# Linear attention with two soft-routed expert layers: VectorE's order in the first chunks, and the first weight loads in pieces of 512 KB

## The reference

```
# attention, per head: B=4, H=8, S=768, D=64
for t in range(S):
    state = gamma * state + outer(k[t], v[t])
    y[t] = scale * (q[t] @ state)
x = y as (3072, 512)                       # N = 3072 tokens, 512 wide
# soft MoE: 8 experts, 4 slots each, F = 1024
logits = x @ phi                           # (N, 32)
d = softmax(logits, axis=0); c = softmax(logits, axis=1)
slot_out[e] = relu((d.T @ x)[e] @ w1[e]) @ w2[e]
x = c @ slot_out
# top-2 MoE, noisy gates
noisy = x @ w_gate + log1p(exp(x @ w_noise)) * noise
out[token] = sum over its two best experts of weight * relu(x @ w1[e]) @ w2[e]
```

## Time and profile before

| | |
|---|---|
| median of 3 runs | 549.07 us (546.41 to 551.51) |
| profiled execution | 547.3 us |
| its span | 545.6 us |
| mean granted TensorE clock | 0.969 |
| PE busy | 496.7 us (91%) |
| DVE busy | 277.1 us (51%) |
| attention, from the start to the first product with w1a | 132.16 us |

### The profile page before, as it was taken

One profiled execution on the slowest core, in us unless ns is written; L12 is line 12 of the kernel. 1 busy time (PEld: TensorE's weight loads), 2 busy tenths in 40 slices (PEclk: granted clock), 3 DMA queues, 4 the chain that ended last, 5 costly groups with the idle time before them and its releaser, 6 DMA issues.

```text
span 545.6 us, 13537 instructions
## 1 busy us (share of the span) xinstructions
PE 496.7 (91%) x4845; PEld 294.6 (54%) x4846; DVE 277.1 (51%) x449; ACT 185.3 (34%) x345; POOL 257.9 (47%) x216
## 2 busy tenths in 40 slices
PE   4898989997977568799999999999999999999995
PEld 4686777873476344345545455454554545545452
DVE  1775757565411698573564645454646242332422
ACT  0121222222000835773645544536352222322210
POOL 1222221212000016455686868686887766656543
PEclk9999999998997688899999999999999999999998
DMA  7999999988999999415554452123232343333410
GB/s 274 358 353 417 373 379 389 336 337 305 420 424 426 403 414 380 165 51 193 188 191 136 125 179 55 30 52 52 36 59 43 47 57 44 47 50 41 55 24 1
DMA packets 32358, 107.91 MB, mean 198 GB/s; under 512 B 11567, under 2 KB 12831, under 8 KB 27840
## 3 DMA queue, kind: packets, MB, share of 16 engines
q1 hardware_dynamic: 18144, 92.89, 44.0%
q0 software_dynamic: 14176, 14.49, 14.7%
HBM read 93.87 MB, written 29.43 MB: 226 GB/s over the span
## 4 chain that ended last, share of the span: by engine, by line
PE 81%; DMA 7%; DVE 6%; issue 3%; ACT 1%; POOL 1%; SPq 0%; DVEq 0%; POOLq 0%
PE ps L988 51%; PE ps L971 5%; PE ps L655 4%; PE ps L719 4%; DMA late_w1a<-chunks 3%; PE ps L861 3%; PE ps L839 3%; DMA w_region<-chunks 3%; PE ps L695 2%; PE ps L709 2%; PE ps L730 1%; PE ps L669 1%; DMA rec_region<-records,idx 1%; PE ps L751 1%; PE ps L922 1%
## 5 line engine op out<-in xcount | busy, mean ns | idle before, releaser
L988 PE MATMUL ps<-w_region,s_region 128*128 (+1 forms) x1320 | 294.9, 380 | 1.1 <-ACT s_region L1177 1.1
L988 PEld LDWEIGHTS ps<-w_region,s_region 128*128 128x128 f16 x1320 | 127.1, 98 | 144.8 <-issue 2.6
L1607 DVE SCALAR_TENSOR_TENSOR s_region<-ps,s_region 128x1024 f16<-128x1024 f32 x55 | 67.4, 1225 | 147.0 <-ACT s_region L1177 147.0
L1177 ACT ACTIVATE s_region<-ps 128x1024 f16<-128x1024 f32 x55 | 56.3, 1024 | 182.3 <-PE ps L971 182.3
L606 POOL DMA_INDIRECT out<-s_region,rec_region x41 | 55.8, 1361 | 52.7 <-DVE s_region L1636 49.9
L612 POOL DMA_INDIRECT out<-s_region,rec_region x42 | 67.9, 1616 | 15.1 <-issue 12.2
L600 POOL DMA_INDIRECT rec_region<-records,idx x55 | 62.0, 1127 | 24.8 <-issue 16.5
L546 POOL TENSOR_TENSOR s_region<-w_region,s_region 128x512 f32<-128x512 f32 x14 | 14.8, 1058 | 51.4 <-PE ps L730 26.7
L971 PEld LDWEIGHTS ps<-s_region,sw_region 128*128 (+1 forms) x440 | 29.7, 99 | 15.7 <-issue 3.0
L1636 DVE TENSOR_SCALAR s_region<-ps,rec_region,y_scale 128x512 f32<-128x512 f32 x42 | 33.8, 805 | 6.5 <-PE ps L988 4.6
L971 PE MATMUL ps<-s_region,sw_region 128*128 128x128 f16 x440 | 34.5, 222 | 1.9 <-ACT sw_region L1130 1.9
(11 more groups left out here) (248 smaller groups left out, 568.8 us busy)
## 6 DMA issues: line engine op xcount, KB each, us to landing
w_region<-moe_w SPq DMA_DIRECT2D x11, 2048.0 KB, 8.6
w_region<-moe_w SPq DMA_DIRECT2D x15, 1024.0 KB, 9.8
w_region<-chunks SPq DMA_DIRECT2D x26, 512.0 KB, 7.3
w_region<-moe_w SPq DMA_DIRECT2D x24, 512.0 KB, 17.2
s_region<-moe_w SPq DMA_DIRECT2D x4, 2048.0 KB, 15.1
sw_region<-chunks SPq DMA_DIRECT2D x12, 512.0 KB, 7.7
late_w1a<-chunks SPq DMA_DIRECT2D x8, 512.0 KB, 8.6
s_region<-moe_w SPq DMA_DIRECT2D x2, 1024.0 KB, 10.9
```

What stands on the lines that cost most here:

```text
L988: last = nc.tensor.matmul(bank[6 + r], h[:, r, f, :], w2b_parts[:, bass.ds(o, 1), part, f, :].rearrange("p e m -> p (e m)"), start=(first ...
L1177: nc.scalar.activation(h_hi[:, r, :, :].rearrange("p c t -> p (c t)").rearrange("p (a n) -> p a n", a=2), ps[:, 2 + 2 * r:4 + 2 * r, :], A ...
L1607: nc.vector.scalar_tensor_tensor(out=h_lo[:, r, :, :].rearrange("p c t -> p (c t)").rearrange("p (a n) -> p a n", a=2), in0=ps[:, 2 + 2 * ...
```

## The change

VectorE's masking of chunk 1's scores moves from ahead of `decay_first(1)` to behind the copies of chunk 0's x and state. The 15 early pieces of w1a of 1 MB become 30 pieces of 512 KB, with a rule that puts one or two behind every chunk from 3 to 23: 1, 1, 2, 1, 2, 1, 2, 1, 1, 2, 1, 2, 1, 2, 1, 1, 2, 1, 2, 1, 2. The bytes, their order and their homes are the same. TensorE's wait ahead of w1a counts 30 pieces instead of 15.

```
+        EARLY_QUARTERS = 4 * (E - 1) + 2
...
-            def w1a_half(e, half):
-                words = slice(half * HALF, (half + 1) * HALF)
-                sp.dma_start(w1a_home[e][:, words], w1a[e, :, words]).then_inc(w1a_early, 16)
-
-            def late_w1a_words(first, last):
-                sp.dma_start(late_w1a[:, first:last], w1a[E - 1, :, first:last]).then_inc(w1a_early, 16)
+            def w1a_quarter(e, q):
+                words = slice(q * UNIT // 4, (q + 1) * UNIT // 4)
+                to = late_w1a if e == E - 1 else w1a_home[e]
+                sp.dma_start(to[:, words], w1a[e, :, words]).then_inc(w1a_early, 16)
...
             for g in range(3, NT):
                 load_qk(g)
                 load_kv(g)
-                more = (g - 2) * (2 * E - 1) // (NT - 3)
-                for half in range(ahead, more):
-                    if half < 2 * (E - 1):
-                        w1a_half(half // 2, half % 2)
-                    else:
-                        late_w1a_words(0, LATE)
+                more = (g - 2) * EARLY_QUARTERS // (NT - 3)
+                for q in range(ahead, more):
+                    w1a_quarter(q // 4, q % 4)
                 ahead = more
...
-            pe.wait_ge(w1a_early, 16 * (2 * E - 1))
+            pe.wait_ge(w1a_early, 16 * EARLY_QUARTERS)
...
                     if c < NC - 1:
                         keep_state(b, c)
+                    if t == 0:
+                        mask_scores(0, 1)
...
             mask_scores(0, 0)
             decay_first(0)
-            mask_scores(0, 1)
             decay_first(1)
```

More of the change, by code:

```diff
@@ L444, in _ @@
             sp.dma_start(ident_stack[:, :], consts[:, ident_at:ident_at + P + SL]).then_inc(ident_full, 16)
-            HALF = UNIT // 2
-            def w1a_half(e, half):
-                words = slice(half * HALF, (half + 1) * HALF)
-                sp.dma_start(w1a_home[e][:, words], w1a[e, :, words]).then_inc(w1a_early, 16)
-            def late_w1a_words(first, last):
-                sp.dma_start(late_w1a[:, first:last], w1a[E - 1, :, first:last]).then_inc(w1a_early, 16)
+            def w1a_quarter(e, q):
+                words = slice(q * UNIT // 4, (q + 1) * UNIT // 4)
+                to = late_w1a if e == E - 1 else w1a_home[e]
+                sp.dma_start(to[:, words], w1a[e, :, words]).then_inc(w1a_early, 16)
             ahead = 0
@@ L468, in _ @@
                     sp.dma_start(gates[:, :, E:2 * E], w_noise.rearrange("(c p) e -> p c e", p=P)).then_inc(small_full, 16)
-            assert ahead == 2 * E - 1
+            assert ahead == EARLY_QUARTERS
             def load_w2b(o):
```

## The result

The changed kernel takes 544.95 us in the median of 20 runs (543.50 to 549.33), the kernel before 547.78 (545.52 to 551.51, 20 runs as well). The ratio is **0.9953, with a 95% interval of 0.9932 to 0.9973**: 2.6 us faster (1.5 to 3.7). The forecast was 2.5 us. The profiled execution has a span of 543.2 us, 2.4 less than before.

A forecast was written before the change was run, and what follows sets the result against it. In the attention TensorE and the DMA engines were taken to stand close together, neither far ahead. VectorE's order 1.3 us plus the spread 1.2 us made 2.5 us, so 549.07 - 2.5 = 546.5 us, range 542.0 to 551.0.

The forecast's parts named there:

- VectorE's order, 1.3 us: At chunk 0, TensorE's 1.32 us wait for VectorE's copy of x goes, since x no longer queues behind chunk 1's masking.
- kv(4) went out at 13.30: In the first chunks, SP issues kv(4) at 14.0 instead of 15.97, when chunk 1's scores are done; earns nothing of itself.
- The rival by which the constants for x held TensorE anyway: At chunk 0, something else holds TensorE until 16.6 us, so part one gives 0: 547.9 us, chance 0.07.
- The spread, 1.2 us: At chunks 8 to 10 and 16 to 17, one piece less queued ahead of late loads wins 0.62 us per run.
- SP's issuing costs 0.43 us or so for each load: On SP in the attention, issuing further loads costs 0.43 us or so each, and SP waits between chunks anyway.
- The price of smaller pieces, 0 to 2.0 us: In the attention's DMA queue, 0.066 us more per 512 KB piece, at most 2.0 us for 30; the lower end is nothing.
- the sign that the prediction named for a price: At chunks 8 to 10, a DMA share of 1.0 with under 400 GB/s would show that smaller pieces cost.
- The loads are the bound: In the attention, loads land when they did and TensorE's 1.3 us return as waits: 549.6 us, chance 0.24.
- All waits go: In the attention, all 4.4 us of waits for loads vanish besides the 1.3 us: 5.7 us won, 543.4 us, chance 0.15.
- A fixed time for each load: In the attention's DMA queue, each of 15 further loads costs a fixed time; at 1.3 us each 555.6 us, chance 0.04.
- The waits down to 3 us, none over 1: In the profile after, TensorE's waits for loads in the attention fall from 4.4 us to about 3, none over 1 us.
- That what follows only shifts: Behind the attention, every stage stays as long as it was, so a microsecond won in the attention is kept.

The follow-up runs named there:

- the repeat: The changed kernel, with both parts of the change, timed again against the kernel before: ratio 0.9965.
- order alone: The kernel before with only VectorE's new order, w1a still in 15 halves, run twice: ratios 0.9967 and 0.9948 to before.
- the pieces alone: The changed kernel with VectorE's old order, w1a in 30 pieces of 512 KB, run twice: ratios 0.9991 and 0.9987 to before.
- before with late gates: The kernel before with only the loads of the gates' weights moved behind the attention: ratio 0.9985 to before.
- 512 KB in the old places: The changed kernel with two 512 KB pieces behind each chunk that had one half before, none behind the others: ratio 0.9964 to before.
- the comparison of halves with spread pieces: VectorE's new order and gates' loads behind the attention, w1a in 15 halves: 0.9965 to before; with spread pieces, 0.9913 (512 KB) or 0.9924 (256 KB).
- 60 pieces: The changed kernel with the gates' loads behind the attention and w1a in 60 pieces of 256 KB: ratio 0.9924 to before.
- the late gates: The changed kernel with the two loads of the gates' weights issued behind the attention instead of behind chunk 6: ratio 0.9913 to before.
- the one with w1a behind: The changed kernel with gates' loads behind the attention and all 30 early w1a pieces issued behind chunk 23's loads: ratio 1.0384 to before.

## Why the prediction was right

**The total was right, and in its split there is luck**: 2.5 us forecast, 2.6 us measured (1.5 to 3.7), and the repeat gave 1.9 us. But order alone gave 1.8 and 2.9 us, as much as both parts together, where the sum had 1.3; the pieces alone gave 0.6 where it had 1.2, with intervals that include nothing. One part measured larger and one smaller than forecast, and they met near the sum. With the gates' rows out of the way it is the other way round: 1.1 us for the order and 2.2 or more for the spread. So the two parts don't simply add up, and how the 2.6 us split between them is not shown.

**VectorE's order, 1.3 us: the mechanism right, the size not settled.** The wait of line 669 for x, 1.32 us in the trace of before, is gone in every trace with the new order. With the old order it was 0.88 in the repeat, 1.79 twice with the pieces alone and 0.35 in the slow start of before with late gates. From the first scores to those of chunk 3 it is 13.2 us instead of 14.4, 1.2 won. The two ratios of the order alone (1.8 and 2.9 us) lie above, with intervals that include 1.3. Part of it may be an idle of 0.74 us ahead of the scores of chunk 4, which the profile puts down to no one: 0.61 and 0.30 in the two further traces with halves and the old order, and none in the traces of the other kernels. I named no such term, and what ends it stays open. kv(4) went out at 13.30, when the scores of chunk 1 were done (13.26), as computed. The rival by which the constants for x held TensorE anyway is out: the wait for them ended at 11.33 us.

**The spread, 1.2 us: the mechanism seen in the traces, its size in the changed kernel not shown.** The step said that the waits behind runs of three halves shrink by one piece's time less the price. At chunks 9 and 10 they went entirely, at 16 and 17 by 0.9 us; with 512 KB in the old places they came back at 10, 16 and 17. But what this won in the changed kernel was partly spent on a wait that I had not foreseen, at chunk 7. Pieces alone are worth 0.6 us or nothing with that hold in the way, and beside the order alone they add nothing that can be seen; with the gates' rows gone, the comparison of halves with spread pieces says 2.2 to 2.8 us. The traces agree: from the scores of chunk 4 to those of chunk 23 the four with the new order and spread pieces take 88.6, 87.0, 86.3 and 86.3 us (the last two with late gates), the four with the new order and halves or the old places 89.3 to 91.8. With the old order and the gates' rows in place there is no such difference: 89.3 and 89.4 us with halves, 89.9 and 89.2 with pieces. So the sum lacked a term, the hold, and 1.2 was too little for the spread without it.

**"SP's issuing costs 0.43 us or so for each load": this step failed.** The issue behind the gates' rows took 2.27 us, 1.66 in the repeat and 2.99 and 2.57 with the pieces alone. The trace of before showed the sign of it, 1.23 us for kv(7), and far behind the attention, among queued loads of 512 KB, one issue of 6.50 us at 178.57. Moving the gates' loads brought the issue back to 0.33 us and the kernel to 0.9913. With halves an issue behind the same rows takes 0.5 to 1.2 us, so what else is queued counts too. The short rows are no condition: the changed kernel has other long issues of chunk loads, with no short rows near:

```profile
66.18 1.52 SPq L419 DMA_DIRECT2D w_region<-chunks  x1
78.68 1.47 SPq L419 DMA_DIRECT2D w_region<-chunks  x1
```

**The price of smaller pieces, 0 to 2.0 us:** the lower end. From 42 to 62 us the changed kernel's loads run at 389 GB/s with a share of 1.00, the sign that the prediction named for a price, and in its repeat at 405, against 411 before; but 60 pieces cost nothing measurable. The upper end rested on a stretch that was not, as it said, of 512 KB loads alone: of the 9.98 MB moved there GpSimd's own transfers were 0.87, with 8.5% of the engines' time.

**The rivals.** "The loads are the bound" would have been 549.6: the slow stretches were slow since little was queued there, as the spread filled them. In single executions the loads do take a lead back, as in the first trace of the order alone. "All waits go" (5.7 us) is near what the late gates give (4.8), but not in the way it says: 2.5 us of waits were left in that trace. "A fixed time for each load" is out by the 60 pieces. "The waits down to 3 us, none over 1" was wrong in the first trace (4.8, one of 1.64) and right in the second (2.3, none over 1).

**That what follows only shifts** does not hold from trace to trace, and no run tests it in the mean. The stage of the products with w1a took one of three lengths over all traces: 16.2 us (the changed kernel, its repeat and four others), 17.8 (before and its repeat, and two others) or 18.4 to 19.0 (four kernels, the fastest among them). It follows the granted clock at its start.

## What to carry to other kernels

When weights are prefetched behind loads that the compute waits for, put the same small amount behind each step instead of a large piece behind some: what counts is how much stands in the queue ahead of the next needed load, and here neither 512 KB nor 256 KB pieces cost anything measurable in a full queue. Try loads of many short rows in another place than such a queue; here that was worth some 2 us, by ratios from different groups, with spread pieces and little or nothing with halves. Look for an issue instruction that takes longer than its neighbours, even by a microsecond. And on an in-order engine, work that waits for a later product goes behind the copies that are ready.

## What the runs showed of the hardware

**With much queued, an issue can take microseconds, and short rows make it longer.** Two loads of 16 KB in 512 rows each made SP's next issues take 1.66 to 2.99 us with 512 KB pieces spread around them, and 0.33 us without them. Elsewhere in the attention of the changed kernel, without short rows, single issues took 1.52 and 1.47 us; in the kernel before, in a stage of queued 512 KB loads, one took 6.50.

**A wait for a load can cost TensorE its clock.** With the pieces alone TensorE waited 2.26 us ahead of the scores at 44.01. Three stretches around it (length, busy time of PE, clock, DMA share, GB/s):

```profile
40.00:44.00 4.00, 1.76 (x34) 1.00 0.99 389
44.00:48.00 4.00, 3.99 (x42) 0.57 1.01 413
48.00:52.00 4.00, 4.00 (x84) 1.00 1.03 413
```

A granted clock of 0.57 in the mean is mostly the lower level, 1.2 GHz. From the scores of chunk 8 to those of chunk 9 it took 6.8 us, against 5.3 in the changed kernel, 1.5 us more than the wait itself. The repeat had the same (clock 0.57, 6.8 us) behind a wait of 1.45 us with two short ones ahead, and so had, to a lesser degree, the 2.06 and 2.05 us waits of the order-only kernel and of the old places (clocks of 0.67 and 0.61). Other waits left the clock at 1.00: the changed kernel's of 1.64 us at chunk 7, that of before of 1.54 at chunk 16, and one of 1.95 at chunk 23 with the order alone. So a late load can cost more than its wait, and need not.

**The same at the start of the products with w1a.** From 126 to 130 us TensorE is busy for 2.0 to 3.0 of 4 us in all traces but the one with w1a behind. The changed kernel kept its full clock through it and needed 16.2 us for the stage; before fell to a mean of 0.70 from 134 to 138 us and needed 17.8; the changed kernel with late gates had 0.50 from 126 to 130 and needed 18.4. This makes some 2 us of scatter between executions, nearly as much as the whole change is worth, and it isn't settled here what decides it.
